# Loading the dense layer's weights through GpSimd's queue and not SyncE's

## The chip, the cores and the metric

The program runs on one core of a Trainium2 chip. The metric is the device time of one execution in microseconds (us), given as the median of several. The traces come from one profiled execution of the program; times in them count from the start of its span. The names of the engines are those of the profile: PE is TensorE, PEld its weight loads, DVE VectorE, ACT ScalarE, POOL GpSimd, SP SyncE.

## What is computed

Three layers stand one after the other, all in 32-bit floats.

```
# 1: attention, batch 2, 8 heads, 768 tokens, head size 64
k_sum, v_sum = max of k and mean of v over blocks of 32 tokens      # 24 summaries a head
scores = [scale * q @ k.T where |i - j| < 16 else -1e9,  scale * q @ k_sum.T + log(32)]
attn   = softmax(scores) @ [v, v_sum]
# 2: dense layer on x = attn as [1536 tokens, 512]
h   = x @ w_in                       # w_in  512 x 2048
g   = where(h > 0, h, exp(min(h, 0)) - 1)
x2  = g @ w_out                      # w_out 2048 x 512
# 3: the best of 8 experts for each token, by normalised dot products
out = gate * (relu(x2 @ w1[e]) @ w2[e])
```

## The kernel before

Each engine has its own program, written out by hand, and the engines meet at semaphores. The 1536 tokens are six blocks of 256. A unit `u` is one block and one pair of heads; there are 24, four to a block. For the first block (units 0 to 3) the attention is done ahead of everything: PE turns keys and queries, makes the scores (`scores`), turns the softmax's rows (`transpose_p`), makes the value means (`means_of_two`) and multiplies by the values (`values`). Then the dense layer starts: `hidden(n)` is x by one eighth of w_in, `project(n)` one eighth of w_out, and between these steps stand the attention pieces of the next blocks (`between`). Every fp32 product is made of three: a high part of each operand, and low parts for what the high part leaves.

The dense layer's weights come in eight parts of each matrix, 512 KB a part. A part of w_in is read in pieces of 1 KB (256 columns), one of w_out in pieces of 2 KB (512 columns). They land in `w_raw`; ACT makes the high parts (`split_high`, L1386 and L1389), DVE the low ones (`split_low`, L1696), and PE reads both during block 0 alone (`hidden`, L976; `project`, L1020 to L1033). The first part of w_in is used by `hidden_of_pair` and `hidden_low` (L991 to L999). The last 1536 columns of `w_raw` hold attention rows of units 1 to 3 until these are done, so the last two parts of w_out must wait for that.

All loads of this stretch stand in one program, SP's. Keys, values and queries are there too. A value window of a unit (`load_windows(u)`, L507 and L511) and a unit's queries (`load_q(u)`, L490) are read in pieces of 256 bytes (64 numbers of one head). Windows of units 0 to 3 are 184 KB each (two of 72 KB and one of 40 KB), of units 4 to 7 192 KB; a unit's queries are 128 KB. `load_windows(u)` for a later unit waits for `o_mm` (its predecessor's values), `load_q(u)` for `q_t` (its buffer's queries turned). These waits hold up all that stands behind them on SP, the weights too.

POOL builds the mask, then for each unit the columns of keys that PE's scores read (`key_columns(u)`, L714 and L717), into two buffers in turn; unit u's copy waits for the scores of unit u - 2 (`s_mm`). Behind `key_columns(5)` it makes constants that are read much later (`constants`, L693 to L702). `kb_ev` tells PE that a unit's columns are there. Until the third layer POOL issues no transfer; there it gathers and scatters rows with indirect ones (L753, L776), 128 rows of 2 KB each.

Of the kernel before, what the change touches and what calls it, by code (L numbers as in the profile page):

```python
# [35 lines left out]
P = 128  # L36
# [4 lines left out]
def build(nc, q, k, v, w_in, w_out, expert_emb, tau, w1, w2, out):  # L41
# [131 lines left out]
    with ExitStack() as ctx:  # L173
# [289 lines left out]
        def w_in_part(w, s):  # L463
            return w[:, s * CHUNK:(s + 1) * CHUNK]

        def w_out_part(w, s):
            return w[:, WIN_SZ + s * 2 * DM:WIN_SZ + (s + 1) * 2 * DM]
# [5 lines left out]
        def _(sp):  # L473
# [11 lines left out]
            def load_q(u):  # L485
                head, tok = heads_of(u)
                if u >= PAIRS:
                    sp.wait_ge(q_t, u - 1 if u >= PAIRS + 2 else u - PAIRS + 1)
                for h in range(2):
                    sp.dma_start(q_source(u).rearrange("p (t n) -> p t n", n=P)[:, :, h * D:(h + 1) * D],  # L490
                                 qh[head + h, tok:tok + TB, :].rearrange("(t p) d -> p t d", p=P)
                                 ).then_inc(ld_q[u % 4], 16)
# [18 lines left out]
                    sp.dma_start(vwin[lo - key0:hi - key0, g, w, :].rearrange("p (h d) -> p h d", h=2),  # L511
                                 vh[head:head + 2, lo:hi, :].rearrange("h p d -> p h d")).then_inc(ld_vw[g], 16)

            def load_w_in(s):
                sp.dma_start(w_in_part(w_raw, s).rearrange("p (c f) -> p c f", c=DC),
                             w_in[:, s * 2 * P:(s + 1) * 2 * P].rearrange("(c p) f -> p c f", p=P)
                             ).then_inc(ld_win[s], 16)

            def load_w_out(s):
                sp.dma_start(w_out_part(w_raw, s).rearrange("p (c n) -> p c n", c=2),  # L520
                             w_out[s * 2 * P:(s + 1) * 2 * P, :].rearrange("(c p) n -> p c n", p=P)
                             ).then_inc(ld_wout[s], 16)

            def store_x2(i):
                sp.wait_ge(acc_a, i + 1)
                sp.wait_ge(acc_d, i + 1)
# [27 lines left out]
            load_v0(2)  # L554
            load_v0(3)
            load_windows(1)
            load_w_in(0)
            load_windows(2)
            load_windows(3)
            load_q(4)  # L560
            load_w_in(1)
            load_w_out(0)
            load_q(5)
            load_w_in(2)
            load_windows(4)
            load_w_out(1)
            load_w_in(3)
            load_windows(5)
            load_w_out(2)
            load_q(6)  # L570
            load_w_in(4)
            load_windows(6)
            load_w_out(3)
            load_q(7)
            load_w_in(5)
            load_windows(7)
            load_w_out(4)
            load_w_in(6)
            load_w_out(5)
            load_w_in(7)  # L580
            load_w_out(6)
            load_w_out(7)
            sp.wait_ge(m_mm, PAIRS)
            sp.dma_start(emb[0:E, :], expert_emb).then_inc(ld_emb, 16)
            sp.dma_start(tau_sb[:, :], tau.to_broadcast([E, 1])).then_inc(ld_emb, 16)
# [67 lines left out]
        def _(pool):  # L653
# [52 lines left out]
            def key_columns(u):  # L706
                j, g = divmod(u, PAIRS)
                if u >= 2:
                    pool.wait_ge(s_mm, u - 1)
                if j % BPB == 0:  # L710
                    pool.wait_ge(k_ev, 2 * PAIRS * (j // BPB) + 2 * g + 2)
                at = j % BPB * TB
                for w in range(WINS):
                    pool.tensor_copy(kb[u % 2][:, w, 0:KW], kT[:, g, at + w * QS:at + w * QS + KW])  # L714
                if j % BPB == 0:
                    pool.wait_ge(kmx, PAIRS * (j // BPB) + g + 1)
                pool.tensor_copy(kb[u % 2][:, :, KW:KC], kmaxT[:, g:g + 1, :].to_broadcast([P, WINS, NSUM])  # L717
                                 ).then_inc(kb_ev, 1)
# [3 lines left out]
            means_matrix()  # L722
            key_columns(2)
            key_columns(3)
            key_columns(4)
            key_columns(5)
            constants()
            key_columns(6)
            key_columns(7)
# [1387 lines left out]
```

## Time and profile before

| | |
|---|---|
| median of 3 runs | 546.83 us (546.75 to 547.37) |
| the profiled execution | 546.45 us |
| its span, first to last instruction | 544.7 us |
| PE busy | 532.5 us, 98% of the span |
| DVE, ACT, POOL busy | 301.7, 234.0, 82.0 us |
| DMA | 49.23 MB; first queue 42.36 MB, POOL's 6.30 MB |
| granted TensorE clock, mean | 0.998 |

Of the 546.45 us of the profiled execution 1.75 lie outside its span. PE's busy time is what fills the span; matmuls are pipelined, so a busy PE is not a PE at its peak. What is left to read are the moments where PE is not busy, and they stand nearly all in the first 28 us. In rows of the timeline, "x4" means four instructions merged, and what stands in brackets is the engine's idle time before them and what ended it. An idle time put down to "issue" is one for which the profile shows no releaser.

### The profile page before, as it was taken

Reading aid. Unit: us, or ns where it says so; the run is one execution under the profiler, and the core shown is the slowest. Engines: PE = TensorE matmul, PEld = TensorE weight load, DVE = VectorE, ACT = ScalarE, POOL = GpSimd, SP = SyncE. Lnnn points to the kernel's source line nnn. Section 1 sums busy time; section 2 is a strip of 40 time slices with the busy share of each in tenths; the row PEclk is TensorE's granted clock in tenths of the full one; section 3 lists DMA queues with packets and bytes.
Section 4 is the critical chain, followed back from the end, with each engine's and each line's share of the span. In section 5 each row is a group of like instructions: output and inputs, shape, how many; then the busy total and the mean of one; then the engine's idle time right before and its main releaser. Section 6 shows DMA issues by size and latency. Waiting matters only on the chain.

```text
span 544.7 us, 11801 instructions
## 1 busy us (share of the span) xinstructions
PE 532.5 (98%) x3930; PEld 458.7 (84%) x3931; DVE 301.7 (55%) x667; ACT 234.0 (43%) x530; POOL 82.0 (15%) x210
## 2 busy tenths in 40 slices
PE   8799999999999999999999999999999999999995
PEld 7688888888888888888889898888788888888883
DVE  3789887544644464447542557667583274322552
ACT  5677764443544453444332436461171251211440
POOL 6312020011100000000000000110312131111221
PEclk9999999999999999999999999999999999999999
DMA  9999322232121112110100720010875155101000
GB/s 208 275 273 315 91 48 64 54 75 71 50 64 24 25 25 64 25 25 15 40 1 2 266 84 0 20 59 2 309 256 185 44 206 188 39 28 35 19 19 24
DMA packets 63499, 49.23 MB, mean 90 GB/s; under 512 B 46038, under 2 KB 52182, under 8 KB 63456
## 3 DMA queue, kind: packets, MB, share of 16 engines
q1 hardware_dynamic: 61056, 42.36, 27.1%
q0 software_dynamic: 2400, 6.30, 3.5%
q8 instruction: 27, 0.44, 0.4%
q14 instruction: 16, 0.13, 0.1%
HBM read 43.40 MB, written 6.82 MB: 92 GB/s over the span
## 4 chain that ended last, share of the span: by engine, by line
PE 97%; ACT 1%; issue 1%; DVE 0%; POOLq 0%; DVEq 0%; ACTq 0%
PE bank L976 25%; PE bank L1020 8%; PE bank L1027 8%; PE bank L1033 8%; PE bank L1188 5%; PE bank L1234 5%; PE bank L1242 5%; PE bank L1196 5%; PE bank L1190 5%; PE bank L1236 5%; PE bank L954 3%; PE bank L936 2%; PE bank L927 2%; PE bank L1226 2%; PE bank L1086 1%; PE bank L832 1%
## 5 line engine op out<-in xcount | busy, mean ns | idle before, releaser
L1395 ACT ACTIVATE el<-bank 128x512 f32<-128x512 f32 x48 | 28.7, 597 | 106.0 <-PE bank L976 105.7
L1700 DVE TENSOR_SCALAR el<-el 128x512 f32<-128x512 f32 x48 | 20.7, 431 | 87.8 <-ACT el L1395 87.8
L976 PE MATMUL bank<-x_hi,w_hi_parts 128*128 128x256 f32 x376 | 60.9, 283 | 0.0
L976 PE MATMUL bank<-x_hi,w_lo_parts 128*128 128x256 f32 x376 | 60.4, 282 | 0.0
L976 PE MATMUL bank<-x_lo,w_hi_parts 128*128 128x256 f32 x376 | 60.2, 282 | 0.0
L976 PEld LDWEIGHTS bank<-x_hi,w_hi_parts 128*128 128x128 f32 x376 | 53.6, 188 | 3.2 <-issue 0.2
L1020 PE MATMUL bank<-w_hi_parts,g_hi 128*128 128x512 f32 x192 | 54.9, 408 | 0.0
L1027 PE MATMUL bank<-w_lo_parts,g_hi 128*128 128x512 f32 x192 | 52.8, 397 | 0.0
L1033 PE MATMUL bank<-w_hi_parts,g_lo 128*128 128x512 f32 x192 | 52.5, 395 | 0.0
L976 PEld LDWEIGHTS bank<-x_lo,w_hi_parts 128*128 128x128 f32 x376 | 51.5, 189 | 0.0
L976 PEld LDWEIGHTS bank<-x_hi,w_lo_parts 128*128 128x128 f32 x376 | 51.3, 188 | 0.0
L714 POOL COPY kb<-kT 128x96 f32<-128x96 f32 x96 | 25.2, 305 | 165.7 <-PE bank L927 141.1
L1188 PE MATMUL bank<-w_hi_parts,xsT_hi 128*128 (+1 forms) x112 | 45.7, 408 | 0.4 <-issue 0.4
L1234 PE MATMUL bank<-w_hi_parts,hT_hi 128*128 (+1 forms) x112 | 44.6, 399 | 0.6 <-ACT hT_hi L1540 0.6
L1190 PE MATMUL bank<-w_lo_parts,xsT_hi 128*128 (+1 forms) x112 | 44.4, 396 | 0.0
L1236 PE MATMUL bank<-w_lo_parts,hT_hi 128*128 (+1 forms) x112 | 44.4, 396 | 0.0
L1033 PEld LDWEIGHTS bank<-w_hi_parts,g_lo 128*128 128x128 f32 x192 | 36.3, 189 | 8.9
L1027 PEld LDWEIGHTS bank<-w_lo_parts,g_hi 128*128 128x128 f32 x192 | 36.1, 188 | 8.6
L1707 DVE TENSOR_TENSOR g_lo<-el,g_hi 128x512 fp32r<-128x512 f32 x48 | 33.1, 690 | 16.0 <-ACT g_hi L1401 16.0
L1401 ACT CAST g_hi<-el 128x512 fp32r<-128x512 f32 x48 | 29.9, 623 | 26.7 <-DVE el L1702 26.7
L1540 ACT CAST hT_hi<-bank 128x512 fp32r<-128x512 f32 x28 | 15.0, 589 | 56.5 <-PE bank L1226 56.5
L1020 PEld LDWEIGHTS bank<-w_hi_parts,g_hi 128*128 128x128 f32 x192 | 32.6, 189 | 4.6 <-issue 0.2
(282 smaller groups left out, 917.6 us busy)
## 6 DMA issues: line engine op xcount, KB each, us to landing
raw<-in_moe_w SPq DMA_DIRECT2D x8, 2048.0 KB, 8.9
w_raw<-in_moe_w_in SPq DMA_DIRECT2D x8, 512.0 KB, 7.4
w_raw<-in_moe_w_out SPq DMA_DIRECT2D x8, 512.0 KB, 7.6
k_raw<-in_k SPq DMA_DIRECT2D x16, 192.0 KB, 3.2
v_raw<-in_v SPq DMA_DIRECT2D x8, 384.0 KB, 4.3
x_rows<-x SPq DMA_DIRECT2D x6, 512.0 KB, 4.1
q_raw<-in_q SPq DMA_DIRECT2D x44, 64.0 KB, 2.9
vwin<-in_v SPq DMA_DIRECT2D x32, 72.0 KB, 2.8
```

The costliest lines, as they stand in the source:

```text
L976: mm = pe.matmul(o, r32(w[:, at:at + P]), r32(x[i % 2][:, c, :]), start=(part == "hh" and c == 0), stop=(part == "lh" and c == DC - 1))
L1020: pe.matmul(bank[:, ACC[t], :], r32(g_hi[n % 2][:, rows(a, t)]), r32(W_HI[:, at:at + DM]), start=(s == 0 and a == 0), stop=False)
L1027: pe.matmul(bank[:, ACC[t], :], r32(g_hi[n % 2][:, rows(a, t)]), r32(W_LO[:, at:at + DM]), start=False, stop=False)
L1033: mm = pe.matmul(bank[:, ACC[t], :], r32(g_lo[n % 2][:, rows(a, t)]), r32(W_HI[:, at:at + DM]), start=False, stop=(s == STEPS - 1 and a == 1))
L1188: pe.matmul(bank[:, H1[a], :], r32(xsT_hi[:, c, :]), r32(W_HI[:, bass.ds(at, 512)]), start=(c == 0), stop=False)
L1190: pe.matmul(bank[:, H1[a], :], r32(xsT_hi[:, c, :]), r32(W_LO[:, bass.ds(at, 512)]), start=False, stop=False)
L1196: mm = pe.matmul(bank[:, H1[a], :], r32(xsT_lo[:, c, :]), r32(W_HI[:, bass.ds(base + (c * F2 + a * 512), 512)]), start=False, stop=(c == D ...
L1234: pe.matmul(bank[:, 4, :], r32(hT_hi[:, f, :]), r32(W_HI[:, bass.ds(at, DM)]), start=(f == 0), stop=False)
L1236: pe.matmul(bank[:, 4, :], r32(hT_hi[:, f, :]), r32(W_LO[:, bass.ds(at, DM)]), start=False, stop=False)
L1395: act.activation(el[n % 2], bank[:, H_BANK[n % 2], :], ACT.Exp).then_inc(e_act, 1)
L1401: act.copy(r32(g_hi[n % 2]), el[n % 2]).then_inc(g_hi_a, 1)
L1707: dve.tensor_tensor(r32(g_lo[n % 2]), el[n % 2], g_hi[n % 2], ALU.subtract).then_inc(g_ev, 1)
```

## The change

The two functions that load parts of w_in and w_out are moved from SP's program to POOL's. SP is left with keys, queries, values and windows, and its order changes a little: the queries of units 6 and 7 now stand ahead of the windows of units 5 and 6. On POOL the first part of w_in stands behind `key_columns(3)`; all others stand behind `key_columns(5)`, and `constants` and `key_columns(6)` behind them. Before the last two parts of w_out POOL waits for `o_mm` of the four first units.

```
-            load_w_in(0)
             load_windows(2)
             load_windows(3)
             load_q(4)
-            load_w_in(1)
-            load_w_out(0)
             load_q(5)
-            load_w_in(2)
             load_windows(4)
-            load_w_out(1)
-            load_w_in(3)
+            load_q(6)
             load_windows(5)
-            load_w_out(2)
-            load_q(6)
-            load_w_in(4)
+            load_q(7)
             load_windows(6)
-            load_w_out(3)
-            load_q(7)
-            load_w_in(5)
             load_windows(7)
-            load_w_out(4)
...
-            load_w_out(7)
             sp.wait_ge(m_mm, PAIRS)
...
             key_columns(3)
+            def load_w_in(s):
+                pool.dma_start(w_in_part(w_raw, s).rearrange("p (c f) -> p c f", c=DC),
+                             w_in[:, s * 2 * P:(s + 1) * 2 * P].rearrange("(c p) f -> p c f", p=P)
+                             ).then_inc(ld_win[s], 16)
...
+            load_w_in(0)
             key_columns(4)
             key_columns(5)
+            load_w_in(1)
+            load_w_out(0)
+            for s in range(2, STEPS - 1):
+                load_w_in(s)
+                load_w_out(s - 1)
+            load_w_in(STEPS - 1)
+            pool.wait_ge(o_mm, PAIRS)
+            load_w_out(STEPS - 2)
+            load_w_out(STEPS - 1)
             constants()
             key_columns(6)
```

On POOL, from the second half of `key_columns(5)` to the first copy of `key_columns(6)`, the rows stood like this before (`kb` are the key columns, `token_less` to `before_r` the constants):

```order
L717 COPY kb<-kmaxT 128x4x24
L693 IOTA token_less 128x12
L695 IOTA rev 128x8 [waits pool_c]
L697 IOTA slot_i 128x24 [waits pool_c]
L699 MEMSET ex 128x8 [waits pool_c]
L700 MEMSET ex 128x8 [waits pool_c]
L701 MEMSET ones_r 128x128 [waits pool_c]
L702 AFFINE_SELECT before_r<-ones_r 128x128 [waits pool_c]
L714 COPY kb<-kT 128x96 [waits pool_c,s_mm]
```

The changed kernel, from the end of `key_columns(3)` (its L688 and L691 are the old L714 and L717, its L667 to L676 the old constants):

```order
L691 COPY kb<-kmaxT 128x4x24 [waits kmx]
L700 DMA w_raw<-in_moe_w_in 128x4x256
L688 COPY kb<-kT 128x96 [waits s_mm]
...
L700 DMA w_raw<-in_moe_w_in 128x4x256
L705 DMA w_raw<-in_moe_w_out 128x2x512
...
L700 DMA w_raw<-in_moe_w_in 128x4x256
L705 DMA w_raw<-in_moe_w_out 128x2x512 [waits o_mm]
L705 DMA w_raw<-in_moe_w_out 128x2x512
L667 IOTA token_less 128x12
...
L676 AFFINE_SELECT before_r<-ones_r 128x128 [waits pool_c]
L688 COPY kb<-kT 128x96 [waits pool_c,s_mm]
```

One transfer of the weights stands between `key_columns(3)` and `key_columns(4)`, and fifteen between `key_columns(5)` and the constants, all ahead of `key_columns(6)`.

On SP, from the windows of unit 2 to those of unit 4, the rows of before were these (`vwin` are the windows, `q_raw` queries):

```order
L515 DMA w_raw<-in_moe_w_in 128x4x256
L507 DMA vwin<-in_v 96x3x64 [waits vw_zero]
L507 DMA vwin<-in_v 96x3x64
L511 DMA vwin<-in_v 80x2x64
...
L490 DMA q_raw<-in_q 128x2x64 [waits q_t]
L490 DMA q_raw<-in_q 128x2x64
L515 DMA w_raw<-in_moe_w_in 128x4x256
L520 DMA w_raw<-in_moe_w_out 128x2x512
L490 DMA q_raw<-in_q 128x2x64 [waits q_t]
L490 DMA q_raw<-in_q 128x2x64
L515 DMA w_raw<-in_moe_w_in 128x4x256
L507 DMA vwin<-in_v 96x4x64 [waits o_mm]
```

In the changed kernel the same stretch holds the small transfers alone:

```order
L507 DMA vwin<-in_v 96x3x64 [waits vw_zero]
L507 DMA vwin<-in_v 96x3x64
L511 DMA vwin<-in_v 80x2x64
L490 DMA q_raw<-in_q 128x2x64 [waits q_t]
L490 DMA q_raw<-in_q 128x2x64
L490 DMA q_raw<-in_q 128x2x64 [waits q_t]
L490 DMA q_raw<-in_q 128x2x64
L507 DMA vwin<-in_v 96x4x64 [waits o_mm]
```

The four weight rows are gone from between them; nothing moved on PE, ACT or DVE.

## Rows read from the trace of the kernel before

**Rows 1.** The page's 40 slices of the span, 13.6 us each: PE, DMA, GB/s.
```profile
PE   8799999999999999999999999999999999999995
DMA  9999322232121112110100720010875155101000
GB/s 208 275 273 315 91 48 64 54 75 71 50 64 24 25 25 64 25 25 15 40 1 2 266 84 0 20 59 2 309 256 185 44 206 188 39 28 35 19 19 24
```
**Rows 2.** Timeline of PE: start, us, engine, line, op, output and inputs, [idle before].
```profile
19.22 1.50 PE L846 MATMUL bank<-v_raw,mean 128*24 128x128 f32 x24 [0.80 <-issue]
...
24.28 0.69 PE L954 MATMUL bank<-pT,vwin 120*64 120x64 f32 x16 [0.90 <-DVE x_lo L1690]
...
26.04 0.69 PE L954 MATMUL bank<-w_raw,vwin 120*64 120x64 f32 x16
...
28.23 0.38 PE L892 MATMUL bank<-ident,q_raw 128*128 128x128 f32 x2
...
33.18 1.18 PE L1020 MATMUL bank<-w_hi_parts,g_hi 128*128 128x512 f32 x4
...
49.71 0.64 PE L927 MATMUL bank<-kb,qT 64*64 64x120 f32 x16
```
**Rows 3.** Timeline of SP's issues, the same columns.
```profile
12.24 0.96 SPq L482 DMA_DIRECT2D v_raw<-in_v  x2
...
14.78 0.45 SPq L515 DMA_DIRECT2D w_raw<-in_moe_w_in  x1
...
17.29 1.21 SPq L511 DMA_DIRECT2D vwin<-in_v  x1
...
19.54 0.46 SPq L511 DMA_DIRECT2D vwin<-in_v  x1
20.05 1.17 SPq L490 DMA_DIRECT2D q_raw<-in_q  x2
...
21.77 0.51 SPq L520 DMA_DIRECT2D w_raw<-in_moe_w_out  x1
```
**Rows 4.** DMA view, windows at these issues in turn: KB each, us to landing.
```profile
v_raw<-in_v SPq DMA_DIRECT2D x1, 384.0 KB, 6.4
...
w_raw<-in_moe_w_in SPq DMA_DIRECT2D x1, 512.0 KB, 7.1
...
vwin<-in_v SPq DMA_DIRECT2D x1, 40.0 KB, 5.6
...
vwin<-in_v SPq DMA_DIRECT2D x2, 40.0 KB, 4.8
...
q_raw<-in_q SPq DMA_DIRECT2D x2, 64.0 KB, 3.3
...
w_raw<-in_moe_w_out SPq DMA_DIRECT2D x1, 512.0 KB, 5.4
```
**Rows 5.** Timeline of POOL.
```profile
15.00 1.40 POOL L714 COPY kb<-kT 128x96 f32<-128x96 f32 x4
...
17.63 0.14 POOL L693 IOTA token_less<- 128x12 f32 x1
...
18.86 0.29 POOL L702 TENSOR_SCALAR_AFFINE_SELECT before_r<-ones_r 128x128 fp32r<-128x128 f32 x1
...
39.99 2.31 POOL L714 COPY kb<-kT 128x96 f32<-128x96 f32 x4 [8.35 <-PE bank L927]
```
**Rows 6.** POOL's gather by line, ns min/median/max; landing times of line L490.
```profile
L753 POOL DMA_INDIRECT xs<-x_rows,token_in x10: 1052/1052/1063, 409.0 to 521.4; - x10
...
DMA to landing us min/median/max: 1.9/2.9/7.1
```
**Rows 7.** Timelines of ACT and then DVE.
```profile
27.99 1.05 ACT L1389 CAST w_hi_parts<-w_raw 128x1024 fp32r<-128x1024 f32 x1
...
31.64 0.62 ACT L1401 CAST g_hi<-el 128x512 fp32r<-128x512 f32 x1 [1.44 <-DVE el L1702]
...
30.39 0.49 DVE L1700 TENSOR_SCALAR el<-el 128x512 f32<-128x512 f32 x1
```

More of the change, by code:

```diff
@@ L512, in load_windows @@
                                  vh[head:head + 2, lo:hi, :].rearrange("h p d -> p h d")).then_inc(ld_vw[g], 16)
[L514 to L522, printed above, removed]
             def store_x2(i):
@@ L560, in _ @@
             load_q(4)
-            load_w_in(1)
-            load_w_out(0)
             load_q(5)
-            load_w_in(2)
             load_windows(4)
-            load_w_out(1)
-            load_w_in(3)
+            load_q(6)
             load_windows(5)
-            load_w_out(2)
-            load_q(6)
-            load_w_in(4)
+            load_q(7)
             load_windows(6)
-            load_w_out(3)
-            load_q(7)
-            load_w_in(5)
             load_windows(7)
-            load_w_out(4)
[L578 to L581, printed above, removed]
-            load_w_out(7)
             sp.wait_ge(m_mm, PAIRS)
@@ L724, in _, with load_w_out @@
             key_columns(3)
+            def load_w_in(s):
+                pool.dma_start(w_in_part(w_raw, s).rearrange("p (c f) -> p c f", c=DC),
+                             w_in[:, s * 2 * P:(s + 1) * 2 * P].rearrange("(c p) f -> p c f", p=P)
+                             ).then_inc(ld_win[s], 16)
+            def load_w_out(s):
+                pool.dma_start(w_out_part(w_raw, s).rearrange("p (c n) -> p c n", c=2),
+                             w_out[s * 2 * P:(s + 1) * 2 * P, :].rearrange("(c p) n -> p c n", p=P)
+                             ).then_inc(ld_wout[s], 16)
+            load_w_in(0)
             key_columns(4)
             key_columns(5)
+            load_w_in(1)
[7 more added lines that the diff above has]
+            load_w_out(STEPS - 1)
             constants()
```

## The prediction, made before the changed kernel had run

> **What bounds the kernel now.** I read the slices of the page first. PE is at 90% or more in all slices but the first, the second and the last, and the DMA engines are full in exactly the first four, up to 54 us, at 208 to 315 GB/s [rows 1]. So the change works in the only stretch where transfers are scarce, and it can win at most what PE idles there because of a transfer. I then read PE's timeline from 15 to 60 us for its gaps. Two of half a microsecond or more stand behind the place where the first weights are issued: 0.80 us before the second group of value means, and 0.90 us before the values of unit 2 [rows 2]. From 28 us on PE has no gap. The 0.80 is a transfer, though the profile names none: SP issues the values of the fourth pair second in the pair of issues that starts at 12.24 and lasts 0.96 [rows 3], so at about 12.7; they land 6.4 us later [rows 4], at 19.1, and PE starts at 19.22 [rows 2]. The 0.90 is put down to DVE, not to a transfer. Weights hold up nothing on PE in this trace. Everything from 28 us on is PE at work, so what is lost before that is lost from the end one for one, and nothing late in the program can give it back.
>
> **Part by part.** *SP's issues.* Sixteen issues leave SP. They cost it about 0.5 us each [rows 3], but no wait of PE hangs on the time at which SP issues: the one transfer that PE waits for is issued ahead of all weights. Gain: 0. Later SP reaches the queries and windows of units 4 to 7 sooner, or behind waits that PE's progress sets; both are used long after. Gain and cost: 0.
>
> *The first part of w_in.* It was issued at 14.78 [rows 3]; now POOL issues it at 15.00, where it began `key_columns(4)` [rows 5], and it reaches the DMA engines one issue later. It used to stand in SP's queue behind the last values and the windows of unit 1. Now it stands in a queue of its own, beside them. The values that PE waits for land at 19.1; the quickest landing of a small load is 1.9 us [rows 6], so their last bytes move until about 17.2. If POOL's descriptors are there at 16.1 (one issue of 1.05 us, the gather's [rows 6]), the two share the engines for the last 1.1 us and the values come up to 1.1 us later; if they are there only after 17.2, no later. I take 0.6, the middle: **0.6 us**, from 0 to 1.1, and PE waits exactly for this.
>
> *The windows and queries beside fifteen more parts.* Before, each of these small transfers stood behind at most the parts that SP had issued ahead. The windows of unit 2 landed at about 17.29 + 5.6 = 22.9, those of unit 3 at 19.54 + 4.8 = 24.3, the queries of unit 4 at about 20.6 + 3.3 = 23.9 [rows 3, 4]; PE reads them at 24.28, 26.04 and 28.23 [rows 2]. So the slack is 1.4, 1.7 and 4.3 us. Now, from about 17.9 on, SP's queue holds the windows of units 1 to 3 and the queries of unit 4, 3 x 184 + 128 = 680 KB in pieces of 256 bytes, and POOL's holds up to two megabytes in pieces of 1 and 2 KB. How the engines divide themselves between the two no row of before shows, since all of this went through one queue. At half the bytes each (145 of 290 GB/s, the mean of two slices' 275 and 273 and one's 315 [rows 1] rounded), the 680 KB take 4.7 us and land at 17.9 + 4.7 + 1.9 = 24.5, long before 28.23: cost 0. At one piece for one piece, a small one waits for a large one each time. Per engine a window is 46 pieces and the queries 32, a part of w_in 32 and of w_out 16. The last window piece is then preceded by about 71 of 1 KB and 16 of 2 KB, 1.65 MB over the engines, and 0.55 MB of its own: 7.6 us, landing at 27.4, against a need at 26.04 + 0.6: 0.8 late. The queries come behind 116 large pieces, 2.37 MB, and 0.68 MB: 10.5 us, landing at 30.3, against 28.23 + 0.6: 1.5 late in all. So this term is 0 to 1.5 us. I take **0.6 us**, a little below the middle, since the parts arrive spaced by their issues and not in one heap.
>
> By the Trainium skill ("DMA: Bandwidth & Descriptors", Queues, rings and completion order) each DMA engine goes round-robin between its queues a packet at a time, not a byte at a time; no row of before shows two queues at once. With small packets on one side and large ones on the other that would be the second reckoning, and the sum would be 2.1 us and not 1.2.
>
> *The weights' own times.* The second part of w_in is issued at 17.63 [rows 5] plus the first part's issue, c, and takes another c. For c = 1.05 it is out at 19.7, the first part of w_out at 20.8, against 21.77 before [rows 3]; the latter landed at 27.2 [rows 3, 4] and ACT read it at 27.99 [rows 7]. So with c up to about 1.5 nothing is later than before, and above it the slack of 0.8 us is used up slowly. Cost 0.
>
> *POOL's other work.* `key_columns(6)` stands behind all of it. It is read at 49.71 [rows 2]. Its start is now 17.63 plus sixteen issues plus the constants, 17.63 to 19.15 = 1.5 us [rows 5], and it takes about 1.3 (two units' columns from 15.00 to 17.63 [rows 5]). It is in time while sixteen issues take up to 49.71 - 17.63 - 1.5 - 1.3 = 29.3 us, 1.83 each. The nearest row is the gather's 1.05 us for 128 pieces [rows 6]; a part of w_in has 512 pieces and of w_out 256. If the price is all per issue, sixteen cost 16.8 us, and the constants and columns are done at 37.2: cost 0. If it is all per piece, they are 4.2 and 2.1 us, 50.4 in all, and PE waits 21.1 us. I take the value near the first end, since the gather also has to read 128 addresses from SBUF: cost 0, with 21.1 as the far end.
>
> The Trainium skill says of this generation ("DMA: Bandwidth & Descriptors", Anatomy of one DMA — SWDGE (gpsimd) path) that many descriptors can be emitted before their number shows in the time; no row has an issue of more than 128 pieces to hold against it. By it the term is 0, as taken.
>
> **The sum.** 0.6 + 0.6 = 1.2 us over the profiled execution's own 546.45 (span 544.7 and 1.75 around it), which gives 547.65; the median of the runs lies 0.4 above that execution, so 546.83 + 1.2 = **548.0 us**.
>
> **The rivals.** *A, the forecast: the small transfers lose their share*, by 0.7 to 2.5 us. For it: the engines are full and two needs stand within 1.7 us of their landings. *B, not slower: the engines divide evenly and POOL's descriptors come late.* The mechanism is the slack itself: with the first part in the engines after 17.2 and half the bytes each, every landing stays ahead of PE's need. It decides as long as the windows of unit 3 land before 26.04. Cost 0 to 0.5, 547.0. For it speaks that weights are not asked of sooner than before. *C, POOL becomes the bound: an issue costs more than 1.83 us on average*, and the scores of unit 6 wait for their columns. At 2.2 us, sixteen take 35.2 and PE loses 35.2 - 29.3 = 5.9 us: 553; at the far end 21.1: 568. For it: four times the gather's pieces; against it: that much of a gather's 1.05 us may be fixed. *D, faster:* the 0.80 us before the value means shrinks, if the weights' pieces, which before were in the same queue, slowed the values that were issued 2 us ahead of them. At most 0.8, 546.0. Against it: the values stood ahead in that queue.
>
> *E, DVE and POOL block each other.* POOL's four copies take 1.40 us at 15.00 and 2.31 at 39.99 [rows 5], beside DVE at work in the second case, so they do disturb each other. An issue of 1.05 us may hold up DVE's minimum of the first hidden step, at 30.39, of which ACT's next cast starts at 31.64 and ends at 32.26 [rows 7] and PE's projection at 33.18 [rows 2]: slack 0.9, so an issue of up to 1.9 us costs up to 1.0. On top of the first term: 546.83 + 0.6 + 1.0 = 548.4. The Trainium skill ("SBUF — State Buffer", Who interferes with whom) has a lock on a port pair that DVE's fast modes and POOL share, and says that descriptor generation starves meanwhile; the stretched copies agree with a lock.
>
> **Chances.** A 0.36, B 0.27, C 0.23, D 0.06, E 0.08. A measurement of this kernel can tell about 0.2%, 1.1 us, from no change. Slower by more: 0.22 of A, 0.22 of C, 0.05 of E, together 0.49. Faster by more: D's 0.8 us does not reach it, so 0.05 for what I have not seen. Within: 0.46. The range is 546.5 to 553.0: below lie D and little else, 0.06, above the dearer half of C, 0.12.
>
> **What the profile of after would show.** The second group of value means starts between 19.2 and 20.3 (first term). The values of unit 3 and the turning of unit 4's queries show idle time put down to a transfer or to "issue" of 0.3 to 1.5 us in all (second term); none there means B. POOL's sixteen issues take about 1.0 to 1.5 us each and its constants are done before 45 us; 2 us or more each and a gap of PE before the scores of unit 6 mean C. DVE's 0.49 us at 30.39 stretched over 1 us means E. From 60 us on both traces should run in step. The prediction is wrong if an issue is dearer than 1.8 us, or if PE's gaps before 28 us get shorter.

## The result, and the profile after

| | before | after |
|---|---|---|
| median | 546.98 us (546.75 to 547.37) | 560.66 us (559.06 to 561.54) |
| profiled execution | 546.45 us, span 544.7 | 559.06 us, span 557.3 |
| PE busy | 532.5 us, 98% | 535.7 us, 96% |
| granted clock, mean | 0.998 | 0.988 |

The ratio is 1.0236, with an interval of 1.022 to 1.0252: slower by 13.7 us, where 1.2 had been forecast and 553.0 was the upper end of the range. The page of the changed kernel, against [rows 1]:

```profile
PE   8786999999999999999999999999999999999994
...
PEclk9987999999999999999999999999999999999999
DMA  9999121222231111110100350010685155100000
GB/s 209 296 350 231 24 47 25 62 62 71 71 101 25 25 25 57 30 24 15 39 1 1 136 205 1 20 58 1 231 303 198 38 191 189 48 27 34 19 19 24
...
q1 hardware_dynamic: 54656, 33.97, 21.0%
q0 software_dynamic: 4704, 14.69, 7.9%
...
PE 90%; DMA 5%; SPq 3%; issue 1%; ACT 0%; POOLq 0%; DVE 0%; DVEq 0%
```

Everything is in slices three and four, 28 to 56 us: PE falls to 8 and 6, the clock to 8 and 7, and the chain that ended last has a transfer in it for 5% of the span. The 8.39 MB of weights moved from q1 to q0, as meant. The first four slices move about as much as before, so bandwidth was not lost. Someone waits for the wrong bytes. PE's timeline of the changed kernel says who; columns as in [rows 2]:

```profile
19.73 1.50 PE L840 MATMUL bank<-v_raw,mean 128*24 128x128 f32 x24 [1.14 <-issue]
...
31.25 0.44 PE L886 MATMUL bank<-ident,q_raw 128*128 128x128 f32 x2 [2.35 <-DMA q_raw<-in_q]
...
32.63 1.08 PE L921 MATMUL bank<-kb,qT 64*64 64x120 f32 x16
...
37.59 0.38 PE L886 MATMUL bank<-ident,q_raw 128*128 128x128 f32 x2
...
49.01 0.69 PE L886 MATMUL bank<-ident,q_raw 128*128 128x128 f32 x2 [5.35 <-DMA q_raw<-in_q]
49.63 1.08 PE L921 MATMUL bank<-kb,qT 64*64 64x120 f32 x16
...
53.12 1.10 PE L1021 MATMUL bank<-w_lo_parts,g_hi 128*128 128x512 f32 x4
...
61.60 0.64 PE L921 MATMUL bank<-kb,qT 64*64 64x120 f32 x16
```

The same instructions before, beside those in [rows 2]:

```profile
29.50 0.64 PE L927 MATMUL bank<-kb,qT 64*64 64x120 f32 x16
...
33.05 0.38 PE L892 MATMUL bank<-ident,q_raw 128*128 128x128 f32 x2
...
38.95 0.38 PE L892 MATMUL bank<-ident,q_raw 128*128 128x128 f32 x2
...
41.25 1.10 PE L1027 MATMUL bank<-w_lo_parts,g_hi 128*128 128x512 f32 x4
```

Subtract one list from the other and the loss has dates. PE is 0.51 us late at 19.73. It is 3.13 late at the scores of unit 4 (32.63 against 29.50), after waiting 2.35 us for their queries. It is 4.54 late at 37.59: no idle time lies between, but scores that took 0.64 us take 1.08. It is 10.06 late at the queries of unit 6, after a wait of 5.35, and 11.87 late at 53.12, again without idle time. From the scores of unit 6 (61.60 against 49.71) it stays 11.9 late, and the spans differ by 12.6. So two waits make 7.7 us, and 1.41 + 1.81 = 3.2 us are lost while PE is busy; the remaining microsecond is the 0.51 of the start and small change. What the spans differ by beyond that stands behind the last scatter's issue: from there to the end it is 3.2 us before and 4.1 after. The table of stretches of the changed kernel says why (busy times by engine, then granted clock, DMA share, GB/s):

```profile
28.00:32.00 4.00, 1.57 (x11) 1.29 (x11) 2.47 (x3) 1.82 (x3) 2.98 (x10) 1.00 1.05 349
...
33.00:34.00 1.00, 1.00 (x17) 0.70 (x10) 0.60 (x2) 0.33 (x1) 0.19 (x1) 0.50 1.10 350
...
36.00:37.00 1.00, 1.00 (x11) 1.00 (x10) 0.97 (x3) 1.00 (x2) 0.00 (x0) 1.00 1.10 347
44.00:49.00 5.00, 0.00 (x0) 0.00 (x0) 1.45 (x3) 2.17 (x3) 0.00 (x0) 0.71 1.05 244
49.00:50.00 1.00, 0.99 (x10) 0.66 (x14) 0.00 (x0) 0.26 (x1) 0.00 (x0) 0.50 0.96 177
```

The granted clock falls to 0.50 (1.2 of 2.4 GHz) twice: at about 32.5 us, when PE had been busy again for 1.2 us after the first idle stretch, and at about 46 us, inside the second. It is back at 1.00 from 36 and from 53 us, with PE busy since 31.25 and 49.01.

Why are the queries late? SP's timeline and the DMA view of 30 to 35 us of the changed kernel (queue, packets, MB, share of 16 engines):

```profile
19.57 1.98 SPq L490 DMA_DIRECT2D q_raw<-in_q  x4
22.47 3.35 SPq L507 DMA_DIRECT2D vwin<-in_v  x2
31.72 1.15 SPq L490 DMA_DIRECT2D q_raw<-in_q  x2
32.92 8.39 SPq L507 DMA_DIRECT2D vwin<-in_v  x2
```
```profile
q0 software_dynamic: 455, 1.62, 93.6%
q1 hardware_dynamic: 455, 0.11, 12.0%
```

In five microseconds each queue moved 455 packets: 1.62 MB of weights in packets of 3.6 KB, and 0.11 MB of queries and windows in packets of 256 bytes. One packet went for one packet, and so the small loads had 7% of the bytes. It stayed like that to 45 us (446 for 446 in the last five). Earlier it was not so: from 20 to 25 us 1368 small packets moved beside 305 of the weights, from 25 to 30 us 632 beside 421. Before, the single queue of the same five microseconds moved this:

```profile
q1 hardware_dynamic: 1695, 1.37, 112.3%
```

868 of those 1695 packets were under 512 bytes. So from 30 us on the small loads move 91 packets a microsecond as long as weights are waiting, and POOL put its last fifteen parts out between 18.84 and 29.80 us, 7.9 MB in 11 us or 717 GB/s, twice what the 16 engines move, so weights were waiting until past 40 us. The queries of unit 6 were issued at 31.72, just after unit 4's had been turned; before it was 29.83 us, so they start 1.9 us later too. The windows of unit 4, 768 packets, stood in front of them, and a small rest of unit 5's queries; with their own 512 these are some 1300 to 1400 packets, 14 to 15 us at that rate, so they would be there at 46 or 47 us. They were there at 49.01. Meanwhile SP itself stood: two issues of windows took 8.39 us.

The rest has another cause. A load raises its semaphore in sixteen steps (I take them to be the shares of the 16 DMA engines), PE waits for the last step, and the trace holds the time of each. Of the 32 steps of unit 6's queries, which are two loads, the first came at 40.9 us, half had come by 44.6 and the last at 49.0; in the kernel before, all came between 35.8 and 37.5. From 46 us on the small loads were no longer slow, with 1590 packets in 3 us beside 37 of the weights, and still the last steps came at 48.5 to 49.0. Of the 32 steps of unit 4's queries half had come by 25.6 and 31 by 28.6, before PE stopped for them at 28.9; the last came at 31.2. The wait of 2.35 us is for this one step. Why one share of a load falls so far behind the others no run here settles.

The Trainium skill ("DMA: Bandwidth & Descriptors", Queues, rings and completion order) says that an engine takes turns between its queues by the packet; with 455 against 455 (packets as the profile counts them) this trace agrees from 30 to 45 us; earlier the counts differ, and no run here says why; whether a turn is one such packet or several, counts over 5 us can't tell.

POOL's own work, against [rows 5]:

```profile
15.17 0.94 POOL L700 DMA_DIRECT2D w_raw<-in_moe_w_in  x1
...
18.84 0.79 POOL L700 DMA_DIRECT2D w_raw<-in_moe_w_in  x1
...
28.38 1.43 POOL L705 DMA_DIRECT2D w_raw<-in_moe_w_out  x2
...
33.81 0.89 POOL L688 COPY kb<-kT 128x96 f32<-128x96 f32 x4 [2.44 <-PE bank L921]
```

An issue costs 0.72 to 0.94 us, and unit 6's columns are made at 33.81, 15 us before even the old kernel needed them.

### The profile page after: what moved, and what is told of

Same layout as the page of the kernel before. It is cut to its first block, busy times and chain, and to the rows that moved or that the text cites. A ratio compares the mean times of both kernels' runs of the same rounds, so it can differ in the third digit from the quotient of the medians.

```text
span 557.3 us, 11801 instructions
## 1 busy us (share of the span) xinstructions
PE 535.7 (96%) x3930; PEld 460.8 (83%) x3931; DVE 301.6 (54%) x667; ACT 233.8 (42%) x530; POOL 91.4 (16%) x226
## 4 chain that ended last, share of the span: by engine, by line
PE 90%; DMA 5%; SPq 3%; issue 1%; ACT 0%; POOLq 0%; DVE 0%; DVEq 0%
PE bank L970 23%; PE bank L1014 8%; PE bank L1021 8%; PE bank L1027 8%; DMA q_raw<-in_q 5%; PE bank L1182 5%; PE bank L1228 5%; PE bank L1236 5%; PE bank L1190 5%; PE bank L1184 5%; PE bank L1230 5%; PE bank L948 2%; PE bank L1220 2%; PE bank L930 2%; PE bank L921 2%; PE bank L1080 1%
## 5 line engine op out<-in xcount | busy, mean ns | idle before, releaser
L688 POOL COPY kb<-kT 128x96 f32<-128x96 f32 x96 | 22.6, 278 | 168.3 <-PE bank L921 143.4
L1228 PE MATMUL bank<-w_hi_parts,hT_hi 128*128 (+1 forms) x112 | 44.6, 399 | 0.6 <-ACT hT_hi L1534 0.6
## 6 DMA issues: line engine op xcount, KB each, us to landing
w_raw<-in_moe_w_in POOLq DMA_DIRECT2D x8, 512.0 KB, 11.4
```

The lines of the kernel that those rows point to most:

```text
L1228: pe.matmul(bank[:, 4, :], r32(hT_hi[:, f, :]), r32(W_HI[:, bass.ds(at, DM)]), start=(f == 0), stop=False)
```

## The experiments

Theory T is that the small loads lose because the queues alternate by packets and POOL's heap of large packets, the weights asked for and not yet moved, is always there. It was set against others: that SP's new order does it, that the first part of w_in does it, that GpSimd's queue is slow in itself, that the lost clock is a cause and not only a consequence.

**two_queues: the disputed cost by itself.** A kernel without the computation. In seven stages it loads one unit's queries in their small pieces (two loads of 64 KB, 512 pieces): alone, behind 4 MB of weights in the same queue, or beside 4 MB from another engine, half of them issued first (shortened):

```
for i in range(n_wide[s]):
    eng.dma_start(dst, src).then_inc(ld_wide[s], 16)   # eng: SP, ACT or POOL
    if i == n_wide[s] // 2 - 1:
        eng.sem_inc(go, 1)                             # SP then issues the small ones
```

> This kernel computes nothing; it leaves out all of the attention and both other layers, writes zeros, and only moves data: 128 KB of queries in 256-byte pieces through SyncE's queue, beside 4 MB of weights through another queue (half of them issued first). Seven stages: the queries alone; behind the 4 MB in the same queue; beside 4 MB from ScalarE's queue in rows of 1, 2 and 4 KB; beside 4 MB from GpSimd's queue, as parts of w_in (four pieces of 1 KB a partition) and as single rows of 2 KB. Theory T (each DMA engine takes one packet from each queue in turn, and GpSimd's transfers go in packets of 4 KB): queries need 32 packets an engine, so with 350 GB/s they land after about 2.5 us alone, 14 behind, 2 + 32 x 1.25 KB x 16 = 3.9 us beside 1 KB rows, 5.4 beside 2 KB, 8.4 beside 4 KB from ScalarE, and the same 8.4 beside w_in from GpSimd although its pieces are of 1 KB. Theory S (a software-made queue starves the hardware queue whatever the sizes): both GpSimd stages over 10 us, all three ScalarE stages near 4. Theory H (only the bytes that are waiting count): all stages beside other queues the same, about 6 to 8.

It ran once, 110.59 us. DVE marks the moment at which the small loads are there; SP's rows show when they were issued (both from this kernel's timelines, each view in a fence of its own):

```profile
31.35 0.06 DVE L92 MEMSET mark<- 128x1 f32 x1 [10.68 <-DMA few_act_one<-in_q]
...
64.31 0.06 DVE L92 MEMSET mark<- 128x1 f32 x1 [12.24 <-DMA few_act_four<-in_q]
...
79.16 0.06 DVE L92 MEMSET mark<- 128x1 f32 x1 [13.08 <-DMA few_pool_four<-in_q]
```
```profile
22.94 1.01 SPq L70 DMA_DIRECT2D few_act_one<-in_q  x2
...
54.02 0.88 SPq L70 DMA_DIRECT2D few_act_four<-in_q  x2
67.80 0.89 SPq L70 DMA_DIRECT2D few_pool_four<-in_q  x2
```

From issue to landing: alone 2.8 us; behind eight parts in SP's own queue 7.5; beside ACT's queue with packets of 1, 2 and 4 KB 8.4, 9.1 and 10.3; beside POOL's with the pieces of w_in 11.4, with one 2-KB piece for each partition 7.3. The middle of a stage with 4-KB packets (58 to 60 us, ACT's queue is q10), and of the one with 1-KB packets (28 to 30 us), in the DMA view:

```profile
q10 hardware_dynamic: 193, 0.72, 90.1%
q1 hardware_dynamic: 188, 0.05, 10.5%
```
```profile
q10 hardware_dynamic: 599, 0.59, 87.6%
q1 hardware_dynamic: 403, 0.10, 22.3%
```

Beside ACT's 4-KB packets the exchange is one for one, 94 small packets a us; beside its 1-KB packets they have two for three and twice the speed. So small loads lose beside a queue that isn't GpSimd's too. But all three theories missed the times. T had 3.9, 5.4 and 8.4 us beside ACT and 8.4 beside POOL's parts, too short and too far apart, and 14 where it was 7.5 behind the parts in the same queue. S had the ACT stages near 4 us and both of POOL's over 10. H had all of them alike, at 6 to 8.

Three things T had not in it. Beside ACT's queue 3.5 to 4 us pass before the first small packet moves (24 to 26 us: 533 packets of ACT's, none of SP's), where alone it is 1.1; beside POOL's it is 2 to 3. Beside POOL's parts the exchange was not one for one at all: from 70 to 72 us 403 small packets moved beside 127 large ones. Half of the small load's 32 steps had come by 72.0 us and 30 by 74.0, and only the last two, at 75.8 and 79.1, make it the slowest stage (25 small packets in all between 74 and 80 us). So the 11.4 us are a late last share again and not the rate. That one comes so late in this stage alone, 3.3 us behind the last but one where it is 0.9 at most beside ACT, leaves it open whether POOL's queue has a part in it. And POOL's pieces of 1 KB went out as packets of 3.7 KB (922 packets for 3.40 MB between 68 and 79 us), where ACT's went as 1 KB each.

**reorder: SP's new order without the second queue.** The weights are issued by SP as before, with unit 6's and 7's queries ahead of the windows of units 5 and 6.

```
             load_windows(4)
             load_w_out(1)
             load_w_in(3)
+            load_q(6)
             load_windows(5)
             load_w_out(2)
-            load_q(6)
...
```

> The kernel before with only the other half of the change: SyncE's queries of units 6 and 7 ahead of the windows of units 5 and 6, the weights still in its queue. Theory T (share of packets between two queues): nothing, 547.0 within 0.6. Theory O (the order on SyncE is what delays the queries): a good part of the 13.7 us, at least 4.

Measured: 548.31 us against 547.31 of the kernel before, ratio 1.0014 (0.9997 to 1.0031). PE waits for no queries. The order has no part in the 13.7 us that this run can tell; at most it costs a few tenths of a per cent. Its trace has a gap of 1.06 us before a projection at 47.30, put down to ACT, and ACT had waited 2.79 us for a part of w_out (to 44.83): with the queries ahead, the weights come later.

**first_only: POOL issues the first part of w_in and nothing else of the weights.**

```
+            pool.dma_start(w_in_part(w_raw, 0).rearrange("p (c f) -> p c f", c=DC),
+                           w_in[:, 0:2 * P].rearrange("(c p) f -> p c f", p=P)).then_inc(ld_win[0], 16)
             key_columns(4)
```

> The kernel before with only the first part of w_in loaded through GpSimd, behind key_columns(3). Theory T: the values of the fourth pair share the engines with it and land 0.3 to 0.4 us later, as in the changed kernel (its idle time before the second value means was 1.14 and not 0.80 us): 547.3, and no idle time before the queries of unit 4. Rival: the loss sits in the first part (it delays all that is small): 3 us or more.

Measured: 546.77 us, ratio 0.999 (0.9976 to 1.0003). The second value means wait 0.79 us, as before. The first term of the prediction, 0.6 us, isn't there, nor the 0.3 to 0.4 us that T expected.

**fill: is the clock a cause?** PE gets ten matmuls of the identity before unit 4's wait and twenty-three before unit 6's, so that it isn't idle there.

```
+                for _ in range({4: 10, 6: 23}.get(u, 0)):
+                    pe.matmul(bank[:, b, first:first + P], ident[:, :], ident[:, :], start=True, stop=True)
                 pe.wait_ge(ld_q[u % 4], 32 * (u // 4) + 32)
```

> The changed kernel with idle matmuls (10 before the queries of unit 4, 23 before those of unit 6, their results overwritten) in the two waits. Theory T with the clock as its second half (waits 2.35 + 5.35 us, and about 3.2 us of half clock behind them): 557.5, clock never below full behind the waits. Rival: the time beyond the waits is not the clock: unchanged, 560.7.

Measured: 558.25 us (554.96 to 559.96), ratio 1.0185. The clock's mean is 0.996 and no slice of the page but the last is below 9, but the waits moved (PE's timeline of this kernel):

```profile
37.13 0.41 PE L888 MATMUL bank<-ident,q_raw 128*128 128x128 f32 x2 [1.24 <-DMA q_raw<-in_q]
...
49.80 0.44 PE L888 MATMUL bank<-ident,q_raw 128*128 128x128 f32 x2 [1.44 <-DMA q_raw<-in_q]
```

With the clock kept, PE comes to unit 5 sooner and waits there, and unit 6's queries still land at 49.8. What the clock had cost in the first stretch goes into the next wait; only the second stretch, behind which nothing waits, is won. From the queries of unit 6 to those of unit 7 it is 9.9 us here and 11.7 in the changed kernel, the 1.8 us of that stretch; the medians are 2.4 us apart, but their runs overlap (559.96 here, 559.06 there). The landing of unit 6's queries sets the time, not PE's speed on the way there.

**q67: the late queries issued early.** The queries of units 6 and 7 get a home of their own (free columns of a key buffer) and are issued right behind those of unit 5, ahead of windows 4.

```
+            if u in (6, 7):
+                return k_raw1[:, (2 * TB if u == 6 else 0):(3 * TB if u == 6 else TB)]
...
             load_q(5)
-            load_windows(4)
             load_q(6)
-            load_windows(5)
             load_q(7)
+            load_windows(4)
+            load_windows(5)
             load_windows(6)
```

> The changed kernel, but the queries of units 6 and 7 get a home of their own (free rows of the second batch's key buffer) and are issued with those of units 4 and 5, ahead of the windows of unit 4; the second batch's first keys then wait until unit 7's queries are turned. POOL's weights are untouched. Theory T (beside POOL's standing queue SyncE's packets go one for one with 3.6 KB packets, about 100 a microsecond in all, in the order of issue): queries of unit 4 are as late as before the edit (idle 2.4), those of unit 6 land near 38 and 7 near 43, ahead of PE's need, so the 5.35 us wait and its 1.8 us of half clock go: 550.5 to 551.5. Theory P (SyncE's queue is stopped as long as POOL's holds anything, until 46 us): nothing won, 560.

Measured: 551.67 us (548.69 to 554.75), ratio 1.0072 (1.0036 to 1.0108). Two waits are left, and the one of unit 6 is gone (PE's timeline of this kernel):

```profile
31.08 0.44 PE L891 MATMUL bank<-ident,q_raw 128*128 128x128 f32 x2 [2.42 <-DMA q_raw<-in_q]
...
37.03 0.44 PE L891 MATMUL bank<-ident,q_raw 128*128 128x128 f32 x2 [0.94 <-DMA q_raw<-in_q]
```

The queues still exchange one for one, 456 packets against 455 from 30 to 35 us. Theory P, SP's queue stopped, is out. The span is 7.3 us shorter than the changed kernel's and the median 9.0: more than half of the loss hangs on when the queries of unit 6 are issued, a thing that the prediction had put at nothing.

**two_deep: a smaller heap.** POOL issues a part only when the last but one before it has landed; its constants and `key_columns(6)` stand ahead of the last five parts.

```
+                if n >= 2:
+                    kind, s = out_of_order[n - 2]
+                    pool.wait_ge((ld_win if kind == "in" else ld_wout)[s], 16)
```

> The changed kernel, but POOL issues a part only when the part two earlier has landed, so its queue never holds more than 1 MB; constants and key_columns(6) stand ahead of the last five. Theory T (a packet for a packet while POOL's queue holds anything): the queue is seldom empty, so small packets still go near 100 to 130 a microsecond; 553 to 559. Theory H (the heap of 7.5 MB is what delays the small loads): 548 or less, and no idle time before the queries of unit 6.

Measured: 555.25 us (552.59 to 555.95), ratio 1.0136. The small loads are free: from 30 to 35 us they moved 1344 packets, three times as many, against 218 of the weights. No wait for queries is left. But the time did not come back, for another reason (PE's, then ACT's timeline of this kernel):

```profile
50.48 2.04 PE L1021 MATMUL bank<-w_hi_parts,g_hi 128*128 128x512 f32 x4 [3.03 <-ACT g_hi L1402]
```
```profile
48.02 1.05 ACT L1390 CAST w_hi_parts<-w_raw 128x1024 fp32r<-128x1024 f32 x1 [3.02 <-DMA w_raw<-in_moe_w_out]
```

Two parts outstanding are too few: from 18.66 to 48.28 us a part is issued each 3.3 us on average, the weights come late, and PE waits for them, with its products at half speed behind it (four in 2.04 us, where 1.10 is usual). The steps of a load stay together here: those of unit 6's queries come between 30.6 and 31.5 us. The value lay where T had put it, by a mechanism that T had not named.

**paced: POOL's queue, SP's timing.** POOL issues all sixteen parts, each when SP reaches the place where it issued that part before (the first function below is SP's, the second POOL's; those for w_out are alike).

```
+            def load_w_in(s):
+                sp.sem_inc(paced, 1)
...
             def load_w_in(s):
+                turn[0] += 1
+                pool.wait_ge(paced, turn[0])
                 pool.dma_start(w_in_part(w_raw, s).rearrange("p (c f) -> p c f", c=DC),
```

> The weights go through GpSimd's queue, but each part is released by SyncE at the place in SyncE's old order where its issue stood (constants ahead of the seventh, key_columns(6) ahead of the tenth part). SyncE's small loads and their waits stand as in the kernel before. Theory T: the weights are asked for a little earlier than before since SyncE is no longer held by a full ring, and while they move small loads share packet for packet; the queries of unit 4 have only one part ahead, so no wait there, those of unit 6 compete with about four parts: a wait of 0 to 3 us, 547.5 to 552. Theory Q (it is GpSimd's queue and not the time): about 560 as in the changed kernel. Theory H (only the heap): 547.

Measured: 547.84 us (547.36 to 549.84), ratio 1.0013 (1.0003 to 1.0023), no wait for queries. From 30 to 35 us the small loads moved 717 packets beside 376 of the weights; the DMA view of this kernel from 35 to 40 us:

```profile
q1 hardware_dynamic: 1876, 0.46, 51.8%
q0 software_dynamic: 175, 0.61, 50.5%
```

The same engine, queue and pieces, and of the 2.36% that the change costs 0.13% is left. SP's own order is the old one here, with unit 6's queries behind the windows of unit 5, which should rather delay them. So what costs is when the bytes are asked for. (The profiled execution is the slowest of the ten, 549.84: PE idles 1.81 us before the second value means in it.)

**split and stretched: packet size, or pace.** In split each part is issued as one-row transfers, 48 issues in all; in stretched the transfers stay whole and POOL does idle memsets between them, so that both ask for bytes about as slowly.

```
+                for c in range(DC):
+                    pool.dma_start(w_in_part(w_raw, s)[:, c * 2 * P:(c + 1) * 2 * P],
+                                   w_in[c * P:(c + 1) * P, s * 2 * P:(s + 1) * 2 * P]).then_inc(ld_win[s], 16)
```

That is split (two transfers for a part of w_out). This is stretched, behind each part of w_in; behind each of w_out stands one memset:

```
+                for _ in range(5 if s else 0):
+                    chain(pool.memset(ones_r[:, :], 1.0))
```

> The changed kernel, with each part of w_in read by POOL as four transfers and each part of w_out as two, so that a transfer has one piece of 1 or 2 KB for each partition; bytes, queue and order are the same. In the changed kernel POOL's packets were 4 KB, whatever the pieces. Forty-eight issues of about 0.54 us (two_queues) in place of sixteen stretch the issues to some 3.3 us for a MB. Theory T (the small loads lose because one of their 256-byte packets goes for one large one): if POOL's packets now have 1 and 2 KB, 1.33 KB in the mean, the small loads move 350 GB/s / 1.6 KB = about 220 packets a us in place of 100; the queries of unit 6 with 1750 packets land 8 us after their issue and not 17, PE waits for no queries: 547.5 to 549. Theory P (what matters is only how fast POOL asks for bytes): this kernel and stretched give the same time. If POOL's packets stay near 3.5 KB (the stage with one 2-KB piece for each partition in two_queues had 3.3 KB), the size was not changed, T gives the value of stretched too, and the two can't be told apart by this run.

> The changed kernel, with its sixteen transfers as they are, but five idle memsets of POOL (0.2 to 0.3 us each) behind each part of w_in and one behind each part of w_out, so that POOL's issues take about 3.3 us for a MB, as in split; the packets stay near 4 KB. Theory T: the heap of large packets is smaller but lasts as long as the issues, to about 44 us, since 315 GB/s is nearly all that the engines move; the small loads go at about 100 packets a us at the worst and faster when the heap is empty between parts; PE still waits for queries, less than the 7.7 us of the changed kernel: 549.5 to 553. Theory P (the pace is all): no waits, 547.5 to 549, as split.

Measured: split 554.04 us (551.18 to 556.28), ratio 1.0111 (1.0075 to 1.0147); stretched 549.0 (548.42 to 549.59), ratio 1.0022 (1.0005 to 1.0038), both against 547.85. The packets of split hardly shrank, 1.67 MB in 555 of them, 3.0 KB: this pair can't tell what their size is worth. Its two kernels ask for bytes at nearly the same pace, and yet not quite. The fifteen parts are asked for from 20.79 to 44.35 us in split, 334 GB/s, and from 18.79 to 44.82 in stretched, 302 GB/s. The DMA views from 30 to 35 us, split and then stretched:

```profile
q0 software_dynamic: 555, 1.67, 94.9%
q1 hardware_dynamic: 412, 0.10, 9.3%
```
```profile
q0 software_dynamic: 441, 1.61, 93.8%
q1 hardware_dynamic: 523, 0.13, 11.8%
```

The engines move about 350 GB/s in this kernel. At 302 the small loads catch up sooner (523 packets against 412 here, 1005 against 792 from 35 to 40 us), as they would if the heap ran empty more often; that pace and not the threefold number of transfers makes this difference isn't shown. In split the loss comes at the next place, unit 7's queries, in its timelines of SP and PE:

```profile
36.40 12.08 SPq L507 DMA_DIRECT2D vwin<-in_v  x4
```
```profile
53.51 0.44 PE L886 MATMUL bank<-ident,q_raw 128*128 128x128 f32 x2 [2.57 <-DMA q_raw<-in_q]
```

From 60 us on PE is 6.3 us late in split's trace: besides this wait and the half clock behind it, 1.07 us before the scores of unit 4, where ACT had waited for a part of w_out. (This execution, 556.28, is the slowest of the four, and 3.6 of the 9.9 us by which its span exceeds that of before stand behind the last scatter's issue.) Stretched has a single wait for queries, of 0.44 us at 39.93. T's range for it began at 549.5, a little too high; the theory that pace is all had both at 547.5 to 549, and it failed for split.

**both: an attempt at a faster kernel.** The first part on POOL, the rest on SP, and the last two loads of values ahead of the first windows, to take away the 0.80 us before the second value means.

```
-            load_windows(0)
             load_v0(2)
             load_v0(3)
+            load_windows(0)
             load_windows(1)
```

> The kernel before with the first part of w_in through GpSimd and, on SyncE, the values of the third and fourth pair ahead of the windows of unit 0. The values that PE waits for then have 184 KB less ahead of them, 0.6 us at 290 GB/s, and the windows of unit 0 land near 18, ahead of their need at 21.2. Idle time before the second value means 0.80 to about 0.2: 546.3 to 546.5, ratio 0.999. Rival (the means are held by something else, since the profile names no releaser): 0.80 stays and nothing is won.

Measured: 548.38 us (546.0 to 550.75), ratio 1.0011 (0.9995 to 1.0027). The values were issued 1.5 us sooner and landed at the same time as before; PE started at 19.36 after a gap of 1.15. So the gap is not set by the bytes in front of these values. It too is one late share: fifteen of the sixteen steps had come by 17.5 us, the last came at 19.27 (before, 18.2 and 19.13), and PE starts 0.09 us behind it in either kernel. The windows of unit 2 now came late as well (a wait of 1.22 us), and unit 6's queries (0.50). No kernel of this study is measurably faster than the one before.

## Why the prediction was wrong

*What bounds the kernel.* Right: all of it happened in the stretch where DMA is full, and what was lost there was never given back (+11.9 us at 61.60, spans apart by 12.6).

*The mechanism.* Right in kind: case A, small pieces that lose their share to large ones, one for one from 30 to 45 us. The prediction gave that case its greatest chance, and then priced it with one step too few and without the spread between the shares of one load.

*The step that failed.* "Later SP reaches the queries and windows of units 4 to 7 sooner, or behind waits that PE's progress sets; both are used long after. Gain and cost: 0." Unit 6's queries can be issued only when unit 4's have been turned, and as those came late, it was 31.72 us and not 29.83. By then the windows of unit 4 stand in the queue, at 91 packets a microsecond. "Long after" was 7.2 us (31.72 to 38.95), enough for the 3.3 us of [rows 4] and not for 17.3. Even before it was not long: issued at 29.83, the last share of these queries came at 37.5, 1.4 us ahead of PE. The step put at nothing cost 5.35 us of waiting and 1.81 at half clock; q67 took this wait out, and its span is 7.3 us shorter. Every transfer that is issued while the heap lasts had to be costed at the new rate, not only those next to the edit.

*The second term, windows and queries, 0.6 of 0 to 1.5.* It measured 2.35 us at unit 4's queries (0 at unit 3's windows). The far end's reckoning, one piece for one piece, had these queries at 30.3, and PE got them at 31.25. That is luck. Half of their steps had come by 25.6, not far from the 24.5 of even bytes, and only the last of 32 was late; nor did the packets go one for one then (1368 small beside 305 large from 20 to 25 us). The reckoning is also not what it says: it lets 116 large pieces go ahead of 170 small ones. With 170 it would have been about 34.5, an estimate by its own 290 GB/s. What it had no term for is the late last share. "The parts arrive spaced by their issues and not in one heap" was wrong too: at 0.72 to 0.79 us an issue they come at twice the rate at which they can move.

*What was not in the sum.* The clock: 1.41 + 1.81 us at half speed after the waits. The trace of before never showed it, since PE had no long gap there. Fill shows that it counts only where no wait follows.

*The first term, 0.6.* Not borne out: 0.79 us in first_only, the 0.80 of before. In the kernels here that gap was 0.79 to 1.81, and 1.01 in reorder, where POOL issues nothing; the changed kernel's 1.14 is within that. The reading behind the term, that the bytes ahead set this landing, is what the run named both speaks against.

*The weights' own times, POOL's other work.* Right: costs 0. An issue takes 0.72 to 0.94 us, far from the 1.83 at which case C would begin, and unit 6's columns were never late. What the Trainium skill says on many descriptors being cheap to emit ("DMA: Bandwidth & Descriptors", Anatomy of one DMA — SWDGE (gpsimd) path) agrees so far: 512 pieces cost 0.79 us, 256 cost 0.72.

*Case E.* It did not come, but its condition was not met: DVE's minimum of the first hidden step stood at 33.37 us, 3.6 behind POOL's last issue, and took 0.43 us (0.49 before, [rows 7]). Beside the issues, at 25.74, DVE's making of a low part took 1.22 us, as it had before. The reading that led to E was thin too, since DVE was at work beside both of the copies that it compares. *Case D* didn't come: no gap got shorter. *Case B*: its own condition, the windows of unit 3 in time, was met, and the kernel was slower all the same, since it looked at too few transfers.

*The marks.* "None from 60 us on" held: both traces run in step there. "0.3 to 1.5 us in all" at unit 3 and 4 did not: 2.35.

Still open: why one share of a load comes later than the others, by 1.0 us at the second value means of the kernel before and by 2.6 at unit 4's queries of the changed one; how much of the loss the packets' size makes, since split's hardly shrank; and why the end behind the last scatter's issue is 3.2 us in one execution and 6.7 in another.

## What to carry to other kernels

From 30 us on the two queues here shared by packets, not by bytes or by need. Before large transfers get one of their own, compare the rate at which the new issuer asks for bytes with what the engines move (here 717 against 350 GB/s); if it is above, recompute every small transfer issued until the heap is gone at the small one's share (here 91 packets, 23 KB, a microsecond), with the issues of the same queue in front of it, and look at which of them are issued late because of a buffer. Then leave room for the last share: a wait ends with the last of a load's sixteen steps, which here came 4.4 us behind the middle one for unit 6's queries and 7.1 in one stage of two_queues. The single queue of before was not in the way: it was the pacing, and giving the second queue the old pacing (paced) left 0.13% of the 2.36%.

## What the runs showed of the hardware

POOL's plain transfers of 1-KB and 2-KB pieces moved as packets of 3.6 KB on average (455 for 1.62 MB), those of 1-KB pieces alone as 3.7 KB (922 for 3.40 MB), where the same transfers from ACT moved as 1-KB packets (599 for 0.59 MB). Beside ACT's busy queue no packet of a small load moved in its first 3.5 to 4 us, beside POOL's in its first 2 to 3, where alone it was 1.1. The sixteen steps by which a load reports can lie far apart: 31 of 32 by 28.6 us and the last at 31.2 for unit 4's queries in the changed kernel, 40.9 to 49.0 for unit 6's, which came from 35.8 to 37.5 before. An issue of 512 pieces cost POOL 0.79 us and SP 0.45 to 0.5. SP itself stood while its small packets crept: two issues in 8.39 us in the changed kernel, four in 12.08 in split, where one costs about 0.5 [rows 3]. PE's granted clock fell to 0.50 at 32.5 us, 1.2 us behind an idle stretch of 2.35, and at 46 us inside one of 5.35, and was 1.00 again from 36 and 53 us; it stayed up in fill, where these stretches held matmuls.
